# A routed mixture-of-experts kernel: scatters of a chunk moved ahead of the additions of the same tile, routing steps one slot sooner, direct waits on the scatters

## What is computed

```
w = softmax(weight_gen, axis=-1)                    # (4, 3584, 8 heads, 7 taps)
x = sum over the 7 taps of w[tap] * x_pad[s + tap]  # 14336 rows of 192
noisy = x @ w_gate + log1p(exp(x @ w_noise)) * noise   # 14336 x 8 experts
top2 = the two largest of a row; g = softmax of the two
out[row] = sum over its two experts e of g_e * (relu(x[row] @ w1[e]) @ w2[e])   # 192 -> 1024 -> 192
```

## Time and profile before

| | |
|---|---|
| median of 3 runs | 1276.92 us (1276.27 to 1281.02) |
| profiled execution | 1270.14 us, its span 1268.3 us |
| busy, share of the span | PE 91%, DVE 68%, POOL 53%, ACT 52% |
| the chain that ended last | PE 41%, POOL 20%, DVE 15%, issue 9%, DMA 8%, ACT 5% |
| group of 8 tiles | 72.2 us (group 4) to 76.0 us (group 9) between ScalarE's copies of the first tiles; the last of them, which ends with the padding rows' stores, 80.95 us |

### The profile page before, as it was taken

The page is one execution under the profiler, slowest core; times in us unless marked ns, Lnnn a source line. Parts: engine busy times, 40 slices in busy tenths (PEclk is TensorE's granted clock), DMA queues, the critical chain, the costliest instruction groups (busy, mean ns, idle before and its releaser), DMA issues.

```text
span 1268.3 us, 35686 instructions
## 1 busy us (share of the span) xinstructions
PE 1149.9 (91%) x12139; PEld 1044.9 (82%) x12139; DVE 864.7 (68%) x1738; ACT 662.0 (52%) x1120; POOL 676.3 (53%) x494
## 2 busy tenths in 40 slices
PE   4766299999999999999999999999998988999996
PEld 2332198998989989998998989899898977999996
DVE  6899189695978959696896969689695632333332
ACT  6774254746556464645546465464645543444442
POOL 1046137385665848566584856648475561333333
PEclk9787599999999999999999999999999998999998
DMA  9996314444353444525344443534424344323312
GB/s 311 264 335 188 114 35 103 87 94 92 61 126 66 101 90 84 111 56 129 60 100 90 93 95 58 125 64 97 89 50 84 60 106 82 48 47 50 49 21 27
DMA packets 110752, 124.80 MB, mean 98 GB/s; under 512 B 11372, under 2 KB 102788, under 8 KB 108928
## 3 DMA queue, kind: packets, MB, share of 16 engines
q0 software_dynamic: 45024, 46.59, 23.2%
q1 hardware_dynamic: 65568, 75.92, 20.7%
HBM read 62.82 MB, written 60.22 MB: 97 GB/s over the span
## 4 chain that ended last, share of the span: by engine, by line
PE 41%; POOL 20%; DVE 15%; issue 9%; DMA 8%; ACT 5%; SPq 1%; DVEq 0%; ACTq 0%; POOLq 0%; PEldq 0%
POOL sorted_rows L388 13%; POOL out_rows L399 8%; PE psum L1106 6%; PE psum L1108 6%; PE psum L1109 6%; PE psum L1089 4%; PE psum L1093 4%; PE psum L1090 4%; PE psum L1092 4%; PE psum L1091 4%; DMA st<-sorted_rows 3%; DVE prod L655 3%; DVE hidden L884 3%; PE psum L1078 2%; PE psum L1018 1%
## 5 line engine op out<-in xcount | busy, mean ns | idle before, releaser
L399 POOL DMA_INDIRECT out_rows<-late,st x238 | 392.6, 1649 | 435.4 <-ACT late L523 307.6
L884 DVE SCALAR_TENSOR_TENSOR hidden<-psum,hidden 128x512 f16<-128x512 f32 x476 | 327.4, 688 | 338.0 <-ACT hidden L512 333.6
L512 ACT ACTIVATE hidden<-psum 128x512 f16<-128x512 f32 x476 | 283.8, 596 | 442.6 <-PE psum L1093 442.6
L1106 PE MATMUL psum<-w2s,hidden 128*128 x1904 | 469.6, 247 | 4.7 <-ACT late L523 4.7
L1108 PE MATMUL psum<-w2s,hidden 128*128 x1904 | 469.6, 247 | 0.0
L1109 PE MATMUL psum<-w2s,hidden 128*128 x1904 | 469.6, 247 | 0.0
L1089 PE MATMUL psum<-xT,w1s 128*128 128x256 f16 x952 | 260.3, 273 | 1.0 <-ACT xT L508 1.0
L1091 PE MATMUL psum<-xT,w1s 128*128 128x256 f16 x952 | 260.3, 273 | 0.0
L1090 PE MATMUL psum<-xT,w1s 128*128 128x256 f16 x952 | 260.3, 273 | 0.0
L1092 PE MATMUL psum<-xT,w1s 128*128 128x256 f16 x952 | 260.3, 273 | 0.0
L1093 PE MATMUL psum<-xT,w1s 128*128 128x256 f16 x952 | 260.2, 273 | 0.0
(11 more groups left out here) (175 smaller groups left out, 1226.7 us busy)
## 6 DMA issues: line engine op xcount, KB each, us to landing
st<-sorted_rows SPq DMA_DIRECT2D x119, 202.0 KB, 3.3
xb<-in_x SPq DMA_DIRECT2D x12, 1344.0 KB
out_rows<-zeros SPq DMA_DIRECT2D x19, 576.0 KB, 8.2
st<-in_moe_w SPq DMA_DIRECT2D x5, 768.0 KB, 9.0
out_rows<-late,st POOLq DMA_INDIRECT x238
wb<-in_weight_gen SPq DMA_DIRECT2D x14, 224.0 KB
w2s<-in_moe_w SPq DMA_DIRECT2D x3, 768.0 KB, 12.8
sorted_rows<-pads SPq DMA_DIRECT2D x9, 202.0 KB
```

Of the source, the lines that this page charges most:

```text
L399: pool.indirect_dma_start(out=out, out_offset=bass.IndirectOffsetOnAxis(ap=xr[t % XB][:, s, D + E:D + E + 1].bitcast(I32), axis=0), in_=yo ...
L512: act.activation(hh[:, 2 * q:2 * q + 2, :].rearrange("p j t -> p (j t)"), psH[q][:, :], ACT.Relu).then_inc(hh_ready, 1)
L884: v.scalar_tensor_tensor(hl[:, hq, :].rearrange("p j t -> p (j t)"), psH[q][:, :], 0.0, hh[:, hq, :].rearrange("p j t -> p (j t)"), ALU.ma ...
L1106: nc.tensor.matmul(o, hh[:, j, hs], hi, start=(j == 0 and s == 0), stop=False, skip_group_check=True)
```

## The change

`add_tile` issues the four scatters of a tile first and then the two additions; the wait for the additions' landing stays at its end. The pieces of `route` stand one slot sooner: the first one (and ScalarE's `softplus_exp`) in slot 31 of the group before, the others at slots 0, 2, 3, 4, 6, 7 in place of 1, 3, 4, 5, 7, 8; `AT_LN`, `AT_GATE` and `AT_RANKS` go from 2, 6, 8 to 1, 5, 7. The function `sent` and the semaphore `rows_sent` are gone; the scatters count on one of two semaphores by the chunk's parity, and SyncE and ScalarE wait for those.

```diff
-ROUTE_AT = (0, 1, 3, 4, 5, 7, 8)
-AT_EXP, AT_LN, AT_GATE, AT_RANKS, AT_COUNTS = 0, 2, 6, 8, 13
+ROUTE_FIRST, ROUTE_AT = SLOTS - 1, (0, 2, 3, 4, 6, 7)
+AT_LN, AT_GATE, AT_RANKS, AT_COUNTS = 1, 5, 7, 13
+SENT = 2 * C * 16
...
                     sp.wait_ge(table_ready, (group + 1) * 3)
-                    sp.wait_ge(rows_sent, group + 2 if group <= SHARED else CHUNKS)
+                    for n in range(group + 1 if group else 0, group + 2):
+                        sp.wait_ge(scattered[n % 2], SENT * (n // 2 + 1))
...
-                        in_=rows[n][:, c, :], in_offset=None).then_inc(scattered, 16)
-
-            def sent(n):
-                pool.wait_ge(scattered, (n + 1) * (2 * C * 16))
-                pool.sem_inc(rows_sent, 1)
+                        in_=rows[n][:, c, :], in_offset=None).then_inc(scattered[n % 2], 16)
 
             def add_tile(t, routed=None, between=()):
+                if between and between[0] == 0:
+                    pool.wait_ge(rows_ready, 4 * (routed + 1))
+                for c in between:
+                    scatter(routed, c)
                 for s in range(TH):
                     pool.wait_ge(yo_ready, t * TH + s + 1)
                     pool.indirect_dma_start(
                         out=out, out_offset=bass.IndirectOffsetOnAxis(ap=xr[t % XB][:, s, D + E:D + E + 1].bitcast(I32),
                                                                       axis=0),
                         in_=yo[t % NB][:, s, :], in_offset=None, compute_op=ALU.add).then_inc(added, 16)
-                if between and between[0] == 0:
-                    pool.wait_ge(rows_ready, 4 * (routed + 1))
-                for c in between:
-                    scatter(routed, c)
-
                 pool.wait_ge(added, (t + 1) * (TH * 16))
                 pool.sem_inc(tile_added, 1)
...
             scatter_all(0)
-            sent(0)
             scatter_all(1)
-            sent(1)
...
-                    if c + SEND_COLS >= C:
-                        sent(routed)
...
-                    act.wait_ge(rows_sent, n - 1)
+                    act.wait_ge(scattered[n % 2], SENT * (n // 2))
...
-                    if slot == AT_EXP:
-                        softplus_exp(n - 1)
...
+                if n < CHUNKS and slot == ROUTE_FIRST:
+                    softplus_exp(n)
...
+            softplus_exp(ALONE - 1)
             copy_x(0)
...
-            routing = iter(())
+            routing = route(ALONE - 1)
+            next(routing)
...
                 if slot < SLOTS * (SHARED + 1) and slot % SLOTS in ROUTE_AT:
                     owed -= next(routing)
+                if slot < SLOTS * SHARED and slot % SLOTS == ROUTE_FIRST:
+                    routing = route(ALONE + slot // SLOTS)
+                    owed -= next(routing)
```

More of the change, by code:

```diff
@@ L214, in build @@
          mixed, squares, gate_split, hi_done, rows_ready, transposed, yT_ready, yT_used, logits_done, lg_read, exp_z,
-         abs_z, u_ready, ln_done, diff_ready, exp_d, mask_ready, ranks_done, ranks_read, scattered, rows_sent,
+         abs_z, u_ready, ln_done, diff_ready, exp_d, mask_ready, ranks_done, ranks_read,
          counts_done, macc_ready, padrow_ready, pads_written, table_ready, vchain) = (sem(n) for n in (
@@ L220, in build @@
              "mixed squares gate_split hi_done rows_ready transposed yT_ready yT_used logits_done lg_read exp_z "
-             "abs_z u_ready ln_done diff_ready exp_d mask_ready ranks_done ranks_read scattered rows_sent "
+             "abs_z u_ready ln_done diff_ready exp_d mask_ready ranks_done ranks_read "
              "counts_done macc_ready padrow_ready pads_written table_ready vchain").split())
         x_loaded = [sem(f"x_loaded{i}") for i in range(2)]
+        scattered = [sem(f"scattered{i}") for i in range(2)]
         w1_loaded, w2_loaded = ([sem(f"{n}_loaded{e}") for e in range(E)] for n in ("w1", "w2"))
@@ L968, in _ @@
             parts, part, start, owed, slot = beside_parts(), iter(()), 0, 0.0, -1
-            routing = iter(())
+            routing = route(ALONE - 1)
+            next(routing)
             def beside():
-                nonlocal part, start, owed
+                nonlocal part, start, owed, routing
                 owed += SLOT_US
                 if slot < SLOTS * (SHARED + 1) and slot % SLOTS in ROUTE_AT:
+                    owed -= next(routing)
+                if slot < SLOTS * SHARED and slot % SLOTS == ROUTE_FIRST:
+                    routing = route(ALONE + slot // SLOTS)
                     owed -= next(routing)
@@ L988, in _ @@
             for t in range(TILES):
-                if t % TPC == 0 and t // TPC <= SHARED:
-                    routing = route(ALONE - 1 + t // TPC)
                 for q in range(PAIRS):
```

## The result

| | before | after |
|---|---|---|
| median | 1276.6 us (4 runs, 1272.45 to 1281.02) | 1362.35 us (4 runs, 1361.83 to 1371.57) |
| profiled execution, its span | 1270.14, 1268.3 us | 1371.57, 1369.7 us |
| granted clock, mean | 0.964 | 0.936 |
| a group of 8 tiles, mean of groups 1 to 10 | 74.40 us | 82.97 us |

The change costs 86 us: ratio 1.069, interval 1.064 to 1.074. The forecast had the sign and the place, and a little over half the size: 1326 us, and 1362 lies above its range. The profiled execution of after is the slowest of its four.

A forecast was written before the change was run, and what follows sets the result against it. TensorE, 91% busy, waits once a group for a load behind GpSimd's row of work. Terms 36.1 - 2 - 2.4 + 12.7 + 5 = +49 us on 1270.14 give 1319.5, plus 6.8 to the runs' median: 1326 us; range 1295 to 1348.

The forecast's parts named there:

- Part 1: Routing a slot sooner: `pos` ready 1.9 us sooner, so GpSimd's scatters start 1.9 us sooner per group.
- Part 4: Softplus in slot 31 ahead of tile 7's result: TensorE waits 1.15 us in slot 0, 12.7 us over 11 groups.
- Part 3: Direct waits of SyncE on the scatters: 0.2 us gained per group, 2.4 us in all.
- Rival 1: Waits for the additions' landing do not hold GpSimd; ordinary load stalls go, 1268 us, faster; chance 6%.
- rival 2: Waits cost, but start to start is near 4.0 us or TensorE does not wait in slot 0; 1288 to 1297 us; 20%.
- Rival 3: GpSimd itself becomes the limit, a group 80 us, kernel 20 us slower than forecast, 1345 us; chance 15%.
- Part 2: Scatters first on GpSimd: three exposed landing waits of 2.48 us per group; last scatters later, sum 36.1 us.
- The replay: GpSimd's row worked out from VectorE's additions for twelve groups: last scatter +1.66 to +6.89 us later, mean 3.0.
- the upper bound: On GpSimd, 4.6 us from the second addition's start to the next instruction; 47 us over the groups.
- the clock: TensorE's lower clock behind longer stalls: 4 of 11 groups at 1.3 us, 5 us, bounds 0 and 14.

The follow-up runs named there:

- e4: Changed kernel with the wait for a tile's additions moved behind the next tile's scatters; measured four times: ratios to before 1.031, 1.013, 1.032 and 1.027.
- e2: Kernel before with only the routing steps one slot sooner, softplus in slot 31 included; ratio to before 1.014 (1.007 to 1.020).
- e9: Changed kernel with four of VectorE's six two-input additions a chunk replaced by products that read PSUM; ratios to before 1.060 and 1.056.
- e5: Changed kernel with ScalarE's softplus of slot 31 behind the result of tile 7; 1361.16 us, ratio to before 1.0645 (1.0614 to 1.0675).
- e8: Changed kernel with 80 added TensorE transposes ahead of each group's first, inside the stall; 1393.68 us, ratio to before 1.080 (1.077 to 1.083).
- after again: The changed kernel, unchanged, measured and profiled a second time; 1367.06 us, ratio to before 1.069.
- e10: Kernel before with scatters of three, three and two columns behind the additions of tiles 1, 2, 3; ratios to before 0.994, then 1.008 and 1.006.
- e4b: Second measurement, on another chip, of the changed kernel with the additions' wait behind the next tile's scatters; ratio to before 1.013 (1.011 to 1.016).

## Why the prediction fell short

**What held.** TensorE is bound once a group by the load, and the load by the row of GpSimd: in after the row is 7.4 us longer and the wait for the load grows with it, and e4 shortens the row again. The scatters of the next three tiles do start behind the landing. Part 1 less Part 4: forecast -0.75 us from copy to `pos`, -0.6 to -0.9 in e2, e4 and e9, where the clock doesn't fall. Part 3: -0.26 us against -0.2, but without the one group of 4.75 us it is -0.12. Part 4 alone: forecast 1.15 us a group (its own rows give 312.22 - 311.11 = 1.11), the wait is 16.1 - 4.7 = 11.4 us over the span, e5 gets 1.06 us a group back. Rival 1 falls with the 104.8 us of new waits, rival 2 with start to start of 4.3 to 5.8. Rival 3 did not decide: its 80 us group was passed because of the row and the clock, while between the groups GpSimd still idles before `pos` (148.8 us in 14 waits, 61.0 of them at the start).

**The step that failed first: the size of the landing, Part 2.** The replay took "337.00+4.35 = 341.35" as the rule for every wait, counted from the start of the second addition. Its evidence were additions that VectorE did not hold. The prediction also says that an addition on GpSimd that starts inside an L820 ends late, and applied this to the additions' own end, but not to their landing. Measured, over eleven groups, 8 waits took 5.76 us and 25 took 4.79. Over 4.35 that is 8 x 1.41 = 11.3 us for the held ones and 25 x 0.44 = 11.0 us for the others, whose cause stays open. The mean of the 33 is 5.03 us, beyond the 4.6 us of the upper bound. By kind of instruction, mean of the ten groups between `pos` and the last scatter:

| us a group | before | after |
|---|---|---|
| scatters | 19.51 | 17.69 |
| additions | 11.20 | 12.25 |
| waits beyond the usual 0.30 | 0.15 | 8.29 |

Three waits were to cost 7.4 and cost 8.3; and where the replay had 2.5 us of them given back by scatters that no longer meet VectorE, the scatters gave 1.8 and the additions, which now meet it, took 1.05. So the row grew by 7.4 instead of 4.9: some 27 us over eleven groups. 11 of them are the held landings, 11 the slow ones, and the last 5 that less of the waits was given back than the replay had.

**The second: the clock.** Forecast 4 of 11 groups at 1.3 us, 5 us in all, with a bound of 14 worked out from stalls of 4.6 us. The stalls are 7.9 us and every one brings the lower clock: first tile 12.65 us against 10.9 where the clock doesn't fall (e2, e4, e9, on other chips; 11.05 in e8) is 1.75 us, and the transposes and what follows them to the copy 0.43; 2.2 x 11 = 24 us, 19 more than forecast. The two misses are not independent: the longer row made the longer stall. The clock's 19 us are more than the 11 of the held landings by themselves. Together they are some 46 us of the 52 by which the profiled executions differ more than forecast (101 against 49).

**The range** took its high end from a landing of 4.6 us, start to start, and a clock cost of 14 us. Both were stretched from rows with short stalls and unheld additions, and the case outside those rows came true: 5.03 us, and 24 us.

## What to carry to other kernels

Before a wait is moved, look at what stands behind it on its engine: here four scatters covered each landing, and an order that starts them sooner left the landing bare three times a group. If a rule says that an instruction ends late, let it run through everything that is counted from that instruction, its landing too; and take a landing's spread from waits that were in the open, not from a few clean ones. And price a longer stall with the clock behind it: a stall of 2.3 us mostly cost itself, one of 8 us cost 2 more.

## What the runs showed of the chip

- A GpSimd DMA instruction that starts inside a two-input VectorE addition (1.75 us) ends late, and what it moves lands as late: where the hold made an addition run 2.99 us, 5.76 and 5.77 us (after, after again) from its start to the next instruction, against 4.37 in e9, where VectorE has two such additions a chunk in place of six and none held. Additions that were not held took 4.79 us beside all six; where those 0.4 us come from was not settled; most of them lie in eight waits of 25.
- The Trainium skill (DMA: Bandwidth & Descriptors, section Anatomy of one DMA — SWDGE (gpsimd) path) gives a fixed 2.0 us for such a DMA. The landings at 436.64 and 449.00 come 1.94 and 1.92 us behind the instruction's end, whether it took 1.57 or 2.99 us, and GpSimd goes on 0.8 us later; they agree with a fixed part that counts from the instruction's end. The eight slow landings of the table don't fit it.
- Chips differ: the kernel before took 1276.6, 1289.5 and 1305.1 to 1305.4 us on them, and on the last two kinds ScalarE stood up to 6.8 us at a time until "remote" (e10, third time), in e4b in the fourth tile of every group, while scatters ran:
```profile
339.46 0.60 ACT L509 ACTIVATE hidden<-psum 128x512 f16<-128x512 f32 x1 [1.12 <-PE psum L1093]
345.62 0.60 ACT L509 ACTIVATE hidden<-psum 128x512 f16<-128x512 f32 x1 [5.56 <-remote]
```
No profile of the kernel before was taken there, and the cause is open. Effects under 2% were readable there in the marks of a group, not in the time.
